# Loop bounds of the next expert loaded earlier on TensorE, and three small VectorE operations issued earlier, in an attention and two-layer mixture-of-experts kernel

## What is computed

```python
B, H, S, D = 4, 8, 768, 64          # 3072 tokens of 512
N, D, E, F = 3072, 512, 8, 1024     # experts: E = 8, hidden size 1024
# attention: 8 global columns, a window of 96; softmax(q k^T / 8 + bias) v  ->  x
# layer 0
e_idx = argmax(x @ w_gate, axis=1)
gate_w = softmax(x @ w_gate)[e_idx];  eom = sigmoid(x @ w_output_gate)
for e in range(E):
    h = relu(x[mask] @ w1[e]);  out[mask] = gate_w * eom[:, e] * (h @ w2[e])
# layer 1
logits = normalise(x) @ normalise(expert_emb).T / tau
for e in range(E):
    h = relu(x[mask] @ w1[e]);  out[mask] = gate_w * (h @ w2[e])
```

## Time and profile before

| | |
|---|---|
| median of 3 runs | 1073.19 us (1070.83 to 1075.48) |
| the profiled execution | 1074.15 us, its span 1071.8 us |
| mean granted TensorE clock | 0.986 of full speed |
| TensorE busy (matmuls) | 1018.7 us, 95% |
| TensorE weight loads | 732.9 us, 68% |
| VectorE busy | 601.2 us, 56% |
| ScalarE busy | 345.3 us, 32% |
| GpSimd busy | 197.9 us, 18% |
| layer 0 | about 222 to 669 us of the span |
| layer 1 | about 669 us to the end |

### The profile page before, as it was taken

One profiled execution on the slowest core, in us unless ns is written; L12 is line 12 of the kernel. 1 busy time (PEld: TensorE's weight loads), 2 busy tenths in 40 slices (PEclk: granted clock), 3 DMA queues, 4 the chain that ended last, 5 costly groups with the idle time before them and its releaser, 6 DMA issues.

```text
span 1071.8 us, 24685 instructions
## 1 busy us (share of the span) xinstructions
PE 1018.7 (95%) x6898; PEld 732.9 (68%) x6898; DVE 601.2 (56%) x2649; ACT 345.3 (32%) x1125; POOL 197.9 (18%) x390
## 2 busy tenths in 40 slices
PE   3999999999989999999999999999999999999994
PEld 3888888887666747675766766776657676676772
DVE  6788888857575676566656566733443334333332
ACT  3777766743222232212222122121222113121111
POOL 1122222222122222222212122211111111111111
PEclk9999999999999999999999999999999999999998
DMA  9965557774141514151515150265515153211110
GB/s 176 230 152 141 148 138 217 276 251 120 41 161 63 190 50 178 41 189 42 186 33 197 33 198 32 58 213 194 194 46 199 42 191 134 101 38 39 40 35 18
DMA packets 123517, 134.63 MB, mean 126 GB/s; under 512 B 82220, under 2 KB 82220, under 8 KB 123312
## 3 DMA queue, kind: packets, MB, share of 16 engines
q1 hardware_dynamic: 93408, 54.42, 19.7%
q10 hardware_dynamic: 22368, 57.75, 15.0%
q0 software_dynamic: 7664, 21.56, 5.6%
HBM read 105.55 MB, written 26.92 MB: 124 GB/s over the span
## 4 chain that ended last, share of the span: by engine, by line
PE 58%; issue 23%; DMA 10%; POOL 5%; DVE 2%; POOLq 1%; ACT 0%; SPq 0%; DVEq 0%; ACTq 0%
PE bank L1529 16%; PE bank L1539 14%; DMA bins<-q_in,sidx 9%; PE bank L1426 9%; PE bank L1468 5%; PE bank L1507 4%; PE bank L1655 3%; PE bank L1635 3%; POOL q_in L833 3%; POOL pad_p L776 2%; PE bank L1442 2%; PE bank L1643 1%; DMA kv<-in_k_dram 1%; POOLq L858 0%; DMA x_g<-bins 0%
## 5 line engine op out<-in xcount | busy, mean ns | idle before, releaser
L1529 PE MATMUL bank<-x_gt,w_sb 128*128 128x128 f32 x1856 | 220.9, 281 | 7.0 <-issue 7.0
L1529 PEld LDWEIGHTS bank<-x_gt,w_sb 128*128 128x128 f32 x1856 | 216.8, 197 | 15.6 <-issue 15.6
L1539 PE MATMUL bank<-w_sb,h_t 128*128 128x512 f32 x464 | 204.3, 592 | 0.0
L776 POOL TENSOR_TENSOR pad_p<-zeros 128x1 f32<-128x1 f32 x159 | 39.8, 250 | 801.0 <-DVE y_two L1336 235.3
L992 ACT ACTIVATE h_t<-bank 128x256 f32<-128x256 f32 x168 | 63.1, 382 | 280.1 <-PE bank L1529 265.9
L1539 PEld LDWEIGHTS bank<-w_sb,h_t 128*128 128x128 f32 x464 | 85.7, 190 | 96.1 <-issue 96.1
L1529 PEld LDWEIGHTS bank<-x_gt,kv 128*128 128x128 f32 x832 | 95.7, 194 | 6.9 <-issue 6.9
L1529 PE MATMUL bank<-x_gt,kv 128*128 128x128 f32 x832 | 97.1, 278 | 2.7 <-issue 2.6
L1539 PE MATMUL bank<-kv,h_t 128*128 128x512 f32 x208 | 91.7, 593 | 0.0
L1331 DVE CAST sidx<-r 128x1 int32<-128x1 f32 x31 | 4.8, 153 | 144.7 <-PE bank L1539 117.1
L1029 ACT ACTIVATE y_two<-y_two 128x512 f32<-128x512 f32 x32 | 20.2, 631 | 195.8 <-DVE y_two L1336 160.3
(11 more groups left out here) (205 smaller groups left out, 1444.4 us busy)
## 6 DMA issues: line engine op xcount, KB each, us to landing
w_sb<-in_moe_w_dram ACTq DMA_DIRECT2D x18, 2048.0 KB, 11.5
kv<-in_moe_w_dram ACTq DMA_DIRECT2D x8, 2048.0 KB, 11.7
x_g<-bins SPq DMA_DIRECT2D x120, 133.0 KB, 2.7
w_sb<-in_moe_w_dram SPq DMA_DIRECT2D x4, 2048.0 KB, 16.0
q_in<-in_q_dram SPq DMA_DIRECT2D x24, 256.0 KB, 4.0
kv<-in_k_dram SPq DMA_DIRECT2D x24, 256.0 KB, 4.7
kv<-in_v_dram SPq DMA_DIRECT2D x24, 256.0 KB, 3.5
kv<-in_moe_w_dram SPq DMA_DIRECT2D x2, 2048.0 KB, 15.5
```

The lines of the kernel that those rows point to most:

```text
L776: return nc.gpsimd.tensor_tensor(pad_p[:, at:at + 1], zeros[:, 0:1], zeros[:, 0:1], ALU.add)
L1529: m_ = T.matmul(banks[k][:, f * P:(f + 1) * P], w1[:, c * FF + at:c * FF + at + P], x_gt[:, c, :], start=(c == 0), stop=(c == KC - 1))
L1539: m_ = T.matmul(banks[4][:, :], h_t[:, c, :], w2[:, c * DM:(c + 1) * DM], start=(c == 0), stop=(c == FC - 1))
```

## The change

Two things. On TensorE the loop bounds of expert e + 1 are no longer loaded between the experts but inside `second_half` of expert e: `MID` ahead of c = 1 and `END` ahead of c = 2, in each half tile of experts 0 to 6 (where an expert has two half tiles, twice). Those of expert 0 are loaded in the middle of tile 1's second product, behind `next_x`, and the wait for the table goes with them. On VectorE, in layer 0, the operation in `y_rows` that needs the ids alone is issued ahead of the wait for the rank, and in `next_scores` the operation on the ids and the running sum `pre1` are issued behind the memset and ahead of the eight dots; none of the three is waited for at once. The number of links is the same.

```diff
-                mid = entry(eng, n, MID, e, EARLY + 2 * e + 1, TILES)
-                end = entry(eng, n, END, e, EARLY + 2 * e + 2, TILES)
+                mid, end = mid_of(eng, n, e), end_of(eng, n, e)
...
-                def chain(ins):
+                def issue(ins):
                     nonlocal no
                     no += 1
                     ins.then_inc(L.link, 1)
+
+                def chain(ins):
+                    issue(ins)
                     dve.wait_ge(L.link, STEP_LINKS * at + no)
...
                 def y_rows(i):
 
+                    ids = pay[:, bass.ds(i, 1), 2 * E:2 * E + 1].rearrange("p o c -> p (o c)")
+                    issue(V.tensor_scalar(r1[:, 1:2], ids, 0.0, OFF, ALU.is_equal, ALU.mult))
                     dve.wait_ge(L.rank, i + 1)
-                    ids = pay[:, bass.ds(i, 1), 2 * E:2 * E + 1].rearrange("p o c -> p (o c)")
                     chain(V.tensor_tensor(cmp1[:, :], banks[6][:, 0:E], hot1[:, :], ALU.mult))
                     chain(V.tensor_reduce(r1[:, 0:1], cmp1[:, :], AX.X, ALU.add))
-                    chain(V.tensor_scalar(r1[:, 1:2], ids, 0.0, OFF, ALU.is_equal, ALU.mult))
...
                     V.memset(pad_v[:, 0:1], 0.0)
+                    ids = pay[:, bass.ds(i + 1, 1), 2 * E:2 * E + 1].rearrange("p o c -> p (o c)")
+                    issue(V.tensor_scalar(r1[:, 4:5], ids, 0.0, None, ALU.is_gt))
+                    issue(V.tensor_tensor(pre1[:, :], pre1[:, :], hot1[:, :], ALU.add))
...
-                    chain(V.tensor_scalar(r1[:, 4:5], ids, 0.0, None, ALU.is_gt))
-                    chain(V.tensor_tensor(pre1[:, :], pre1[:, :], hot1[:, :], ALU.add))
...
-                second_full(L, 1, w2, lambda: next_x(L, 2))
+                mids, ends = {}, {}
+
+                def first_bounds():
+                    next_x(L, 2)
+                    pe.wait_ge(L.table, 1)
+                    mids[0], ends[0] = mid_of(pe, n, 0), end_of(pe, n, 0)
+
+                second_full(L, 1, w2, first_bounds)
                 if n == 0:
                     rank_rows(L, 1)
-                pe.wait_ge(L.table, 1)
...
-                def second_half(i, w2):
+                def second_half(i, w2, e):
 
                     pe.wait_ge(L.y, i + FIRST)
                     for c in range(FC // 2):
+                        if c == 1 and e + 1 < E:
+                            mids[e + 1] = mid_of(pe, n, e + 1)
+                        if c == 2 and e + 1 < E:
+                            ends[e + 1] = end_of(pe, n, e + 1)
                         if c % 2 == 0:
                             pe.wait_ge(L.h, PIECES * i + (c // 2 + 3 + FIRST))
...
-                for e, start, mid, end in expert_spans(pe, n):
+                end = EARLY
+                for e in range(E):
+                    start, mid, end = end, mids[e], ends[e]
```

More of the change, by code:

```diff
@@ L574, in expert_spans, with mid_of, end_of @@
             for e in range(E):
-                mid = entry(eng, n, MID, e, EARLY + 2 * e + 1, TILES)
-                end = entry(eng, n, END, e, EARLY + 2 * e + 2, TILES)
+                mid, end = mid_of(eng, n, e), end_of(eng, n, e)
                 yield e, start, mid, end
                 start = end
+        def mid_of(eng, n, e):
+            return entry(eng, n, MID, e, EARLY + 2 * e + 1, TILES)
+        def end_of(eng, n, e):
+            return entry(eng, n, END, e, EARLY + 2 * e + 2, TILES)
         SUPER = STEPS // 2
@@ L1363, in next_scores @@
                     neg = y_row[:, DM:DM + E]
-                    ids = pay[:, bass.ds(i + 1, 1), 2 * E:2 * E + 1].rearrange("p o c -> p (o c)")
                     chain(V.tensor_tensor(neg, dot[:, :], emb_inv, ALU.mult))
@@ L1671, in _ @@
                         h_turn(i, 1)
-                        second_half(i, w2)
+                        second_half(i, w2, e)
                         if n == 0:
```

## The result

The changed kernel takes 1050.2 us (median of 4 runs, 1049.81 to 1050.51) against 1072.6 us for the kernel before beside it; the ratio is 0.9774, with a 95% interval of 0.9755 to 0.9794. The ratio puts the gain at 24 us or 2.3% (the two medians differ by 22.4 us), where 17.9 us were forecast: the direction and the places were right, and the gain was underestimated. The profiled execution took 1050.22 us, its span 1048.1 against 1071.8 us.

The account below looks back on a forecast made before the run. TensorE, busy 95% of the span, was taken as the bound, with idle time and clock falls in the first expert layer. 7.7 + 8.0 + 4.9 - 0.4 - 2.0 - 0.3 = 17.9 us off 1073.19 gave 1055.3 us, range 1049 to 1064.

Parts of the forecast that it names:

- A: Ends of experts, first layer: bounds loaded earlier take each of seven ends from 1.59 to 0.49 us, 7.7 us gained.
- B: Five falls of the granted clock behind experts' ends in the first layer go, 8.0 us gained; bounds 3 to 9.
- C: First layer's half tiles: three operations leave VectorE's chain to `hot1`, 0.45 us less per half tile, 4.9 us together.
- D: Loads inside half tiles cost TensorE 0.3 us each: 0.4 us lost in the first layer, 2.0 in the second.
- E: First bounds, moved into tile 1's second product: 0.3 us lost in first layer, 0 in second.
- rival "slower": Loads not covered at all stop TensorE in 19 half tiles, the clock falls there too: about 1083 us, chance 0.05.
- Rival 1: The clock still falls at some experts' ends, half of B lost: 1059.3 us, chance 0.17.
- rival 2: VectorE's part gives nothing: dots move back and GpSimd's copy of y catches another dot; about 1059 us, chance 0.12.
- the sixth fall: Clock fall after the longest wait for `hot1` (1.8 us); its slow half tile hides the next wait, so counted as nothing.

Follow-up runs that it names:

- one bound left: TensorE's part alone, but with one of the two bounds (MID) loaded between the experts again: 1064.8 us in one run.
- VectorE's part alone: Kernel before with only VectorE's operations moved, bounds still loaded between the experts: 1062.9 us, ratio 0.9922.
- TensorE's part alone: Kernel before with only the bounds loaded inside the half tiles, VectorE as before: 1055.6 us against 1071.05, ratio 0.9857.

## Why the prediction came out as it did

What each part gave in the two profiled executions (spans 23.7 us apart), beside the forecast:

| part | forecast | measured |
|---|---|---|
| A, ends of experts in layer 0 | 7.7 | 9.2 (seven ends, 11.2 to 2.0 us) |
| B, clock | 8.0 | 9.3 (what is left of the 23.7) |
| C, wait for `hot1` | 4.9 - 0.4 | 6.7 (10.1 to 3.4 us) |
| D, layer 1 | -2.0 | 0.0 |
| E, first bounds | -0.3 | 0.0 (1.1 saved, 1.1 lost) |
| attention, untouched | 0 | -1.5 |
| sum | 17.9 | 23.7 |

The attention stage ended 1.5 us later in the profiled execution of after; in the profiles of the other runs, the changed kernel's own second one among them, it ended within 0.5 us of before, so this is spread between executions and not the change.

**Right.** The loads as the bare cost at the ends of the first layer alone, the five falls of the clock as a consequence of both kinds of idle time, VectorE's chain as the path in the half tiles, the second layer untouched by VectorE's part. All falls went, as forecast in part B. The rival "slower" would have needed loads that wait for an empty array; the first load is issued together with the products of c = 0. (That rival's price is added up wrongly: 1073 + 9.9 + 4 + 27 less parts A and C is 1101 us, not 1083.) Rival 1 did not come about with both parts in, but it is what happened with one bound left behind and with VectorE's part alone. What rival 2 feared came about, GpSimd's copy caught another dot (1.09 us), but it no longer ended behind the dots, and the two together gained 0.13 us.

**Wrong, in size: every term to the same side.** The terms A, C and D were each too low by 1.5 to 2.2 us, B by 1.3.

Part D failed in the step "Its pace is bounded by 7.39 / 128 = 0.058 us each, so they are out 0.46 us after 620.62". That was an upper bound of the pace, taken from an array-bound stretch, and then used as the value. Loads at +0.62 (one) and +1.26 us (two) behind the first weights leave nothing for the eight instructions. With that the forecast's own arithmetic gives 0: 0.65 us of load under 0.91 of work, twice. It also took 0.1 us at each end of layer 1 as the price of the loads there; it is still there without them.

Part A failed in the choice of the row. The last expert's end, with 0.49 us, also holds a transition into the next layer; a plain end takes 0.28. So one load is (1.59 - 0.28) / 2 = 0.65 us and not 0.55. The Trainium skill's figure (DMA: Bandwidth & Descriptors, Latency and other measured facts: about 600 ns) was nearer than the forecast's estimate, by the size of the whole `value_load` of 0.64 to 0.67 us. The trace agrees only with that sum: the TENSOR_LOAD alone takes 0.30 us in it, and the register operation, the assertion and the steps between make up the rest.

Part C failed in reading the chain from starts to starts. 616.81 - 616.62 is the time from the removed operation to the next; what goes when it is taken out is the time from the operation ahead of it, 0.51, less what an ordinary link costs, 0.19. The 0.16 us of idle time stood in the rows shown. The price ahead of the dots was twice the one taken (0.27 for 0.13), within its bounds; both errors together left 0.1 us per tile. A second step failed in the overlap: "the copy effectively ends a fixed time after the dots". In the first half tile of a pair the copy left the path, which gave 0.13 us more; in the second it ran among the dots already before. The corrected account is thus 0.69 and 0.56 us. The measured 0.67 in the first half tile of a pair (8.53 to 7.86) and 0.54 in the second (298.79 to 307.74 before, 299.71 to 308.12 after) stand against 0.45. Seven of the eleven waits were of 0.70 to 0.75 us, and they vanished, but for the last one (0.35 us), instead of leaving 0.25.

Part B failed in "I count nothing" for the sixth fall. Its half tile took 1.5 us more (5.14 us for 3.67), and the two waits for `hot1` of that pair, 1.78 and 0 us, sum to hardly less than the 0.70 and 1.27 of another pair: the slow tile hid no waiting on balance, and its removal gave the 1.5 us. The five others gave 7.9.

That the time came out at the very edge of the range has the same reason: the range ruled out that all terms would come out at their better ends together, yet three of them rested on the same habit, of adding a margin against the change at each step.

## What to carry to other kernels

In this kernel a register load on TensorE's sequencer is a stall of 0.65 us for what is issued behind it on that engine, and costs nothing where that much work is queued: put it behind queued work and ahead of the next wait on another engine, not behind that wait. Read the price of an operation in a chain from the end of its predecessor, idle time included. And look at the clock behind short stalls of TensorE: in layer 0 the stalls themselves were 20 us, and the falls they brought on cost 9 more.

## What the runs showed of the hardware

How often the granted clock fell behind the seven ends, by what stood there (a fall is a full tile of over 9 us to its second product, where 7.7 is usual):

| kernel | wait for `hot1`, then time to the first product | falls |
|---|---|---|
| before | 0 to 1.27 us, then 1.58 to 1.67 | 5 of 7 |
| VectorE's part alone | 0 to 1.03, then 1.55 to 1.61 | 3 of 7 |
| one bound left | 0.70 to 1.29, then 0.91 to 0.95 | 3 of 7 |
| TensorE's part alone | 0.70 to 1.28, then 0.28 to 0.31 | 0 of 7 |
| both | 0 to 1.03, then 0.28 to 0.33 | 0 of 7 |

Falls to 0.6 to 0.7 of the clock (1.2 GHz in most of the stretch) cost 1.4 to 1.6 us each, one 2.9. In the three kernels with loads left at the ends, wait and gap together were 1.19 to 1.32 us at nine ends, and two of them were followed by a fall; at twelve they were 1.80 to 2.50 us, and nine were. So a stall of TensorE cost its length here and, with some chance, 1.6 us more. What decides between falling and not at the same gap was not tested.

GpSimd's scatter takes 1.01 us, or about 1.5 where the first dot of VectorE starts 0.06 us ahead of it; its copy of y 0.60 us alone and 1.09 beside dots, and a dot 0.69 or 1.09. The Trainium skill (SBUF — State Buffer, SBUF: two separate sides) says that a vector operation with two inputs in SBUF and a GpSimd operation that reads SBUF exclude each other; the lengthened copy and dots agree with it. The scatter, an instruction that starts a transfer, is held up as well.
